# Second expert's first layer read raw behind the first rows and rounded by ScalarE; two batches scattered in three rounds each, directly behind the mask

## The reference

```python
for t in range(S):
    state = alpha[:, :, t, :, None] * state + np.einsum('bhd,bhe->bhde', k[:, :, t], v[:, :, t])
    y[:, :, t] = np.einsum('bhd,bhde->bhe', q[:, :, t], state)
# x = y as (3072, 384)
expert_idx = np.argmax(logits, axis=1)          # logits = xn @ en.T / tau
for e in range(E):                              # 8 experts, 384 -> 1024 -> 384
    h = np.maximum(x[mask] @ w1[e], 0.0)
    out[mask] = gate_w[mask, None] * (h @ w2[e])
# then x @ w_in (384 -> 2048), ELU, @ w_out (2048 -> 384)
```

## Time and profile before

| | us |
|---|---|
| median of 3 runs | 896.37 (896.36 to 900.02) |
| profiled execution, its time | 898.46 |
| its span | 896.8 |
| TensorE busy | 870.6 (97%) |
| VectorE busy | 435.2 (49%) |
| ScalarE busy | 324.8 (36%) |
| GpSimd busy | 285.7 (32%) |

### The profile page before, as it was taken

How to read it: one execution, slowest core, us unless ns; L and a number is a source line. 1 busy time by engine, 2 the same in 40 slices (tenths; PEclk the granted TensorE clock), 3 DMA queues, 4 the chain that set the end, 5 groups by cost and what they waited for, 6 DMA issues and landing times. The chain is left out here.

```text
span 896.8 us, 16120 instructions
## 1 busy us (share of the span) xinstructions
PE 870.6 (97%) x5725; PEld 777.6 (87%) x5725; DVE 435.2 (49%) x827; ACT 324.8 (36%) x711; POOL 285.7 (32%) x278
## 2 busy tenths in 40 slices
PE   8999999898999999999999999999999999999996
PEld 6888887787899899899888989999999899999985
DVE  7889898851222222223235545445445445445442
ACT  4576667632222222222232223333223233323222
POOL 3235655437455764474708202002002002002001
PEclk9999999999999999999999999999999999999998
DMA  9977774478897888846717002002002002000000
GB/s 151 165 140 137 165 153 113 182 258 282 260 313 249 257 273 264 264 113 206 203 38 243 20 1 71 0 1 72 1 1 71 1 1 71 1 0 27 10 1 35
DMA packets 140974, 107.91 MB, mean 120 GB/s; under 512 B 103354, under 2 KB 129074, under 8 KB 140898
## 3 DMA queue, kind: packets, MB, share of 16 engines
q0 software_dynamic: 25696, 66.09, 23.3%
q1 hardware_dynamic: 115202, 40.79, 20.6%
HBM read 89.51 MB, written 17.35 MB: 119 GB/s over the span
## 5 line engine op out<-in xcount | busy, mean ns | idle before, releaser
L1446 POOL DMA_INDIRECT out<-of,idi x24 | 26.7, 1113 | 365.0 <-ACT of L1552 301.8
L1262 PE MATMUL bank<-WX,hdTh 128*128 (+1 forms) x496 | 128.7, 340 | 0.5 <-PEq L443 0.5
L1488 PE MATMUL bank<-xT_h,wi_h 128*128 128x512 f32 x288 | 114.1, 396 | 0.0
L1488 PE MATMUL bank<-xT_l,wi_h 128*128 128x512 f32 x288 | 113.6, 394 | 0.0
L1488 PE MATMUL bank<-xT_h,wi_l 128*128 128x512 f32 x288 | 113.3, 394 | 0.0
L1580 DVE TENSOR_SCALAR em<-ee 128x512 f32<-128x512 f32 x96 | 44.9, 468 | 135.9 <-ACT ee L1558 134.7
L1558 ACT ACTIVATE ee<-bank 128x512 f32<-128x512 f32 x96 | 57.5, 599 | 146.0 <-PE bank L1488 144.1
L1246 PE MATMUL bank<-WX,xdTh 128*128 (+1 forms) x372 | 101.7, 409 | 4.5 <-POOL WX L1180 3.7
L1180 POOL TENSOR_TENSOR WX<-raw_w,WX 128x3072 fp32r<-128x3072 f32 x14 | 95.4, 6817 | 29.1 <-DMA WX<-moe_w 19.5
L1561 ACT ACTIVATE g_h<-gg 128x512 fp32r<-128x512 f32 x96 | 60.6, 631 | 115.7 <-DVE gg L1585 114.0
L1589 DVE TENSOR_TENSOR g_l<-gg,g_h 128x512 fp32r<-128x512 f32 x96 | 68.2, 710 | 60.2 <-ACT g_h L1561 59.3
(11 more groups left out here) (214 smaller groups left out, 1445.4 us busy)
## 6 DMA issues: line engine op xcount, KB each, us to landing
WX<-moe_w POOLq DMA_DIRECT2D x14, 1536.0 KB, 10.9
raw_w<-moe_w POOLq DMA_DIRECT2D x14, 1536.0 KB, 8.7
xd<-sorted_x SPq DMA_DIRECT2D x31, 193.0 KB, 5.9
sorted_y<-yd SPq DMA_DIRECT2D x31, 192.5 KB, 4.3
xg<-sorted_y SPq DMA_DIRECT2D x6, 770.0 KB, 4.5
nat_a<-alpha SPq DMA_DIRECT2D x32, 144.0 KB, 3.8
nat_k<-k SPq DMA_DIRECT2D x32, 144.0 KB, 3.5
nat_q<-q SPq DMA_DIRECT2D x32, 144.0 KB, 4.2
```

Of the source, the lines that this page charges most:

```text
L1262: last = pe.matmul(y_out(t)[:, 0:DM], hdT[a][:, k * P:(k + 1) * P], WX[:, bass.ds(off + (b * WE + KD * F + k * DM), DM)], start=(k == 0 an ...
L1488: last = pe.matmul(bank[4 + i % 2][:, :], a[:, k, w], b[:, k, :], start=(k == 0 and m == 0), stop=(k == KD - 1 and m == 2))
```

## The change

Batches 0 and 1 scatter twice in each of their rounds 3, 4 and 5, directly behind M1 and ahead of Za: rounds 7, 8, 9 and 11, 12, 13. SP loads only the first expert's first layer before the rows of tiles 0 and 1; the second layer's raw load is issued behind these rows, and behind it, once DVE has subtracted the first layer (s_w at 1), the raw load of the second expert's first layer into the buffer that is then free. ACT rounds it in two halves (upper_copy), one behind Re1 of tile 0, one behind Re1 of tile 1. POOL no longer issues loads for that layer and subtracts when these copies are done.

```diff
-                elif b < PARTIAL - 1 and r == 3:
-                    out_ += [("SC", b * C + j) for j in range(HC)]
-                elif b < PARTIAL - 1 and r == 4:
-                    i = place_of(out_, "M1")
-                    out_[i:i] = [("SC", b * C + j) for j in range(HC, C)]
+                elif b < PARTIAL - 1 and 3 <= r < 6:
+                    i = place_of(out_, "M1") + 1
+                    out_[i:i] = [("SC", b * C + j) for j in range(2 * r - 6, 2 * r - 4)]
...
+        def upper_copy(ac, i):
+
+            if i == 0:
+                peA.wait(ac, "Tq0", PAIRS - 1)
+                ac.wait_ge(s_raw1[0], 16)
+            cols = slice(i * KD * F // 2, (i + 1) * KD * F // 2)
+            ac.activation(parts_of(1)[0][:, cols], raw[0][:, cols], ACT.Copy).then_inc(s_up, 1)
+
         def lower_part(po, e, x):
             upper, lower = parts_of(e)
             cols = W12[x]
-            po.wait_ge(s_raw[x], 16 * e)
-            po.wait_ge(s_hi[x], 16 * e)
+            if (e, x) == (1, 0):
+                po.wait_ge(s_raw1[0], 16)
+                po.wait_ge(s_up, 2)
+            else:
+                po.wait_ge(s_raw[x], 16 * (e - 1 + x))
+                po.wait_ge(s_hi[x], 16 * (e - 1 + x))
...
             e = expert_at(po, 1)
-            for x in range(2):
-                upper_load(po, 1, e, x)
-                raw_load(po, e, x, s_raw)
+            upper_load(po, 1, e, 1)
+            raw_load(po, e, 1, s_raw)
...
             e = expert_at(sp, 0)
-            for x in range(2):
-                raw_load(sp, e, x, s_raw0)
+            raw_load(sp, e, 0, s_raw0)
+            second = expert_at(sp, 1)
             rows = [sp.snap(e * REGION + t * P) for t in range(EARLY)]
             for b in range(PARTIAL):
                 sp.wait_ge(s_scat[b], 16 * C)
             for t in range(EARLY):
                 load(t, rows[t])
+            raw_load(sp, e, 1, s_raw0)
+            sp.wait_ge(s_w, 1)
+            raw_load(sp, second, 0, s_raw1)
...
-            d(("Re1", 0), ("He0", 0), ("He1", 0), ("Re0", 1), ("Re1", 1), ("He0", 1), ("He1", 1))
+            d(("Re1", 0))
+            upper_copy(ac, 0)
+            d(("He0", 0), ("He1", 0), ("Re0", 1), ("Re1", 1))
+            upper_copy(ac, 1)
+            d(("He0", 1), ("He1", 1))
```

More of the change, by code:

```diff
@@ L254, in build @@
         s_raw0 = [sem(f"s_raw0_{x}") for x in "12"]
+        s_raw1 = [sem("s_raw1_1")]
+        s_up = sem("s_up")
         s_raw = [sem(f"s_raw{x}") for x in "12"]
```

## The result

| | kernel before | changed kernel |
|---|---|---|
| median of 4 runs each, us | 898.19 (896.36 to 900.42) | 907.11 (906.34 to 907.82) |
| ratio | | 1.0096 [1.0077, 1.0115] |
| profiled execution, its time | 898.46 | 906.61 |
| its span | 896.8 | 904.8 |
| TensorE busy | 870.6 (97%) | 871.1 (96%) |

The changed kernel is slower by 8.9 us in the medians and by 8.2 us in the two profiled executions. The forecast was +11.1. Its 907.5 lies nearer to the 907.11 than the terms deserve, and that is luck: 1.8 us of it is the median of before, which was 896.37 over three runs and is 898.19 over four.

A forecast was written before the change was run, and what follows sets the result against it. TensorE, busy 97% of the span, was taken as the bound. Masks -1.1, two stops +15.8, experts' start +1.5 and tile 4's release -5.1 summed to +11.1 us on the 896.37 median: 907.5 us, range 902 to 912.

The forecast's parts named there:

- the place and the kind of the loss: Rounds 9 and 13: ScalarE's copy into the batch buffer waits some 8 us for late scatters; TensorE idles about 6.5 us.
- The stops' sum: Rounds 9 and 13: two stops at ScalarE's copy, 7.9 us each, +15.8 us together.
- The landing: Last scatter of rounds 9 and 13: 4.2 us from issue to landing, from twelve earlier scatters at 3.7 to 5.7.
- sentence on the empty queues: Rounds 9 and 13: with the queues empty the last scatter lands as fast as the row loads, 2.4 us.
- The clock: TensorE behind a stop in rounds 9 and 13: half clock, if it comes again, costs 1.4 us.
- the experts' start: First expert tiles: the late second-layer load delays ScalarE's rounding and Gq, +1.5 us, bounds -1.0 to +3.5.
- The wait for the rows: First two tiles: rows come 1.1 to 2.1 us earlier; half of TensorE's 1.7 us wait counted, 0.9 us gained.
- tile 4: Second expert's first layer: GpSimd subtracts earlier, so TensorE's 3.7 us wait and 1.4 us of half clock go, -5.1 us.
- masks at no price: Rounds 8 and 12: mask ahead of the scatters saves 0.57 us each, -1.1 us; nothing taken for scatters before Zm.
- The roots: Round 13: batch 2's roots on GpSimd come 2 us later, hidden under the stop; without it VectorE pays 2 us.
- Short landings: Rival, chance 0.08: last scatter lands in 2.4 us, stops of 6.1 us each, sum +6.0, 902.4 us.
- The other side: Rival, chance 0.05: ScalarE's copy is not held long; with no stop the kernel takes -4.7 us, 891.7.

The follow-up runs named there:

- e5: Changed kernel with a third buffer for a batch's attention output, waits going to the batch three back: 899.24 us, ratio 0.9986.
- e9: Changed kernel with the scatters of rounds 9 and 13 at the head of the round instead of behind the mask: 896.96 us, ratio 0.997.
- e4: Changed kernel with three scatter rounds for batch 0 only; batch 1 scatters three at its round 3's end, three behind round 4's mask: 904.04 us, 1.0045.
- e3: Changed kernel with three scatters at the end of a batch's round 3 and three directly behind round 4's mask: 891.99 us, ratio 0.992.
- e7: e3 with the raw load of the first expert's second layer moved back ahead of the rows: 891.79 us, ratio 0.992.
- e1: Changed kernel with the scatters of the kernel before, so the raw loads alone: 895.06 us, ratio 0.9938.
- e2: Kernel before with only the scatter lines of the change, loads as before: 914.82 us, ratio 1.016.
- e6: Kernel before with e3's scatters and the first expert's second-layer load behind the rows; second expert's weights loaded by GpSimd as before: 897.8 us, 0.9986.
- b0: The kernel before, unchanged, run for a trace on the second chip: 898.22 us.
- e10: e7 once more, unchanged, on the third chip: 897.09 us, ratio 0.9966.

## Why the prediction was right, and where its sizes were off

**Right: the place and the kind of the loss.** The mask alone ends after the time at which the copy would start, then two issues and a landing follow. ScalarE idles 6.8 us before L969 twice with a scatter as releaser, TensorE stops between the halves of the q transposes, 1.0 us behind the copy's start (0.9 forecast). e5 (no wait, no stop), e9 (earlier place, no stop) and e4 (one batch, one stop) show it from three sides. The stretched first issue (2.38, forecast 2.41, ending 0.8 us behind the scan) and the 0.30 between issues came as worked out.

**The stops' sum was right by luck, two errors that cancel.** Forecast 15.8, measured 15.6. The landing was mis-sized: 2.9 us where I took 4.2, lower than any of the twelve of the earlier trace rows. The prediction's own sentence on the empty queues pointed to this, and I still went by rows taken under traffic: DMA share 0.90 over 89 to 99 us of the kernel before, and 0.18 in the stop of round 13. That the traffic is the reason fits these rows; no run varies it alone. The Trainium skill ("DMA: Bandwidth & Descriptors", Anatomy of one DMA) gave 2.5; its estimate is 0.4 under the measured 2.9, my value 1.3 above it. The clock was mis-sized the other way: between nothing and the 1.4 us of one stretch of 3.5 us I took 0.9 a stop; the half clock came at both stops, lasted 6.8 us each, and cost 1.4 and 2.7. With the landing at 2.9 and the clock as measured the working gives 5.7 + 1.4 and 5.7 + 2.7, that is 15.5. Two slips of the working change nothing in this: by its own terms the bounds of a stop are 7.0 - 0.5 = 6.5 and 7.0 + 1.1 + 1.4 = 9.5, not 6.4 and 9.2.

**Wrong: the experts' start, +1.5 forecast, -0.7 measured.** This is the step that carries most of the 3.1 us between +11.1 and +8.0. The forecast had Wc end at 177.0, Re0 behind it, Gq 1.7 us late. In the trace the load took 7.2 (7.8 taken), and it was issued 1.1 us earlier than thought: at 179.24, which less the 13.9 is 165.3, against the 166.4 of the working. Together that is 1.7 us, and Gq's delay came as 0.1. The wait for the rows was sized wrong as well: the working counted half of the 1.7 us of idling and nothing for the half clock behind it, which cost TensorE 4.18 - 2.83 = 1.35 us more. Both are gone. Against them stand the waits for the rounded rows (1.1 us) and for Re0 (1.7), so TensorE is ready for tile 2 only 0.2 us earlier. Its rows come 0.6 us earlier, since the last scatter landed in 3.0 us instead of 3.6, and TensorE no longer waits the 0.4 for them. e3 and e7 show that the place of this load is worth no more than some tenths in the medians of one chip.

**Right: tile 4.** -5.2 against -5.1: the subtraction starts 1.9 us behind GpSimd's first issue, forecast 1.7, at 208.21 - 13.9 = 194.3, forecast 196.2, and both the 3.7 us wait and the half clock are gone. e1, e2 and e6 separate it: it goes with the new way of the second expert's first layer and not with the scatters or with the later load of the second layer.

**Right in the changed kernel, wrong in general: masks at no price.** -1.2 came (forecast -1.1). e3 shows that the same order with three scatters instead of two loses 0.9 of it at Zm. The prediction had looked at Zm and found play enough, for two. On the first and the third chip the same order gained nothing that a profile shows.

**The roots.** The 2 us named for GpSimd's roots without cover came as 2.02 us in e5, and with a stop in round 13 they cost nothing, as round 14's 9.80 against 10.09 shows.

**Rivals.** Short landings was nearer in the landing (2.4 against 2.9), and its two stops were still 3.4 us too small in sum, most of it clock. The other side named 4.7 us of gain for a kernel with no stop; e3, which has none, is 7.2 us faster by the medians and 6.0 between its profiled execution (892.21) and that of b0 on the same chip. The experts' start, -0.7 in place of +1.5, less the 0.9 given back at Zm, covers the 6.0; the distance to 7.2 is in no trace.

**The best version** found is the mask first in two rounds with the raw loads of the change, the second layer early (e7) or late (e3): 0.992 of the time before, 891.8 and 892.0 against 899.14, where the changed kernel has 1.0096.

## What to carry to other kernels

When a producer's last pieces are moved to a later round, look for the consumer of the buffer that they free, and compare two times: the issue of the last piece plus its landing, and the consumer's start. Here the mask's end already lay behind the copy's start, and e9 shows that the same two scatters ahead of the mask cost no stop. Size a landing by rows in which the queues are as full as they will be at the new place, and give an idle TensorE its clock as well, since the same 5.8 us of idling cost 7.2 once and 8.5 once. Read the granted clock behind the waits of the kernel before, too: behind a wait of 1.7 us stood another 1.35 us that the list of waits didn't show.

## What the runs showed of the hardware that I had not expected

- Half clock lasted 6.8 us behind the stops of 5.8 us idle, and 3.4 us behind the gap of 3.2 us in the earlier trace rows. Whether it begins within the idle time or at its end differs between two stops of equal length.
- Half clock came behind shorter idling as well, and not each time: behind 1.7 us in the kernel before (from 170.7) and 2.4 us in e5 (from 160.1), but not behind the 1.7 us of the changed kernel at 188.2 to 189.8, nor behind the 1.9 us of e7.
- The mask, too, is stretched by a scan beside it: 2.20 us at 93.19 and 2.15 at 138.22 in the changed kernel, against 0.86 free of one (147.57); it ends 0.7 us behind the scan of 92.97 to 94.73, as the scatters do. Here it costs nothing.
- The same program has rounds of other length on another chip: 9.4 us in round 8 of e7, 10.7 in round 8 of e10, which is the same kernel. Each is one profile; the other profiles of these chips agree with them.
